# One core, attention feeding two expert layers: a new order of the front's queues, and its first fold row in plain fp32

## The reference

```python
# shortened; softmax stands for exp(s - max) / (sum + 1e-9)
def _attn_ref(x, state):                       # x (8, 8, 512, 64), state (8, 8, 32, 64)
    scores = scale * np.matmul(x, state.transpose(0, 1, 3, 2))
    a = softmax(scores)
    xread = np.matmul(a, state)
    scores2 = scale * np.matmul(state, x.transpose(0, 1, 3, 2))
    a2 = softmax(scores2)
    sread = np.matmul(a2, x)
    return np.concatenate([xread, sread], axis=2)
def _moe_ref(x, w1, w2, w3, w_out):            # d_model 512, d_ff 1024
    return ((x @ w1) * (x @ w2) @ w3) @ w_out
def _moe2_ref(x, w_in, w_out):                 # d_ff 2048
    h = x @ w_in
    return (h - np.tanh(h)) @ w_out
```

## Time and profile before

| | before |
|---|---|
| median of 3 runs | 1281.3 us (1281.1 to 1281.44) |
| profiled execution: its own time | 1281.57 us |
| its span, first to last instruction | 1279.8 us |
| PE busy | 1258.4 us, 98% of the span |
| PEld busy | 1015.4 us, 79% |
| DVE busy | 775.4 us, 61% |
| ACT busy | 555.0 us, 43% |
| POOL busy | 16.0 us, 1% |
| front: `scores(1)` starts | 20.22 us |
| front: `s1(0)` starts | 105.86 us |
| ys starts | 130.91 us |

### The profile page before, as it was taken

The page is one execution under the profiler, slowest core; times in us unless marked ns, Lnnn a source line. Parts: engine busy times, 40 slices in busy tenths (PEclk is TensorE's granted clock), DMA queues, the critical chain, the costliest instruction groups (busy, mean ns, idle before and its releaser), DMA issues.

```text
span 1279.8 us, 17464 instructions
## 1 busy us (share of the span) xinstructions
PE 1258.4 (98%) x6772; PEld 1015.4 (79%) x6772; DVE 775.4 (61%) x1269; ACT 555.0 (43%) x1034; POOL 16.0 (1%) x14
## 2 busy tenths in 40 slices
PE   8998999999999999999999999999999999999998
PEld 7777877777777777788888888888888888888887
DVE  6675244433333434678767677676676776776766
ACT  6675234323333333455444444444444344444443
POOL 0110000000000000000000000000000000000000
PEclk9999999999999999999999999999999999999999
DMA  9850200000000013212100100101001001010000
GB/s 376 309 188 1 83 1 33 34 1 34 34 1 33 34 34 115 66 50 67 50 1 17 50 9 9 50 18 49 0 16 49 0 17 49 16 35 7 8 34 17
DMA packets 17326, 63.77 MB, mean 50 GB/s; under 512 B 1904, under 2 KB 3056, under 8 KB 12656
## 3 DMA queue, kind: packets, MB, share of 16 engines
q1 hardware_dynamic: 16928, 62.59, 13.5%
q10 hardware_dynamic: 336, 0.33, 0.1%
HBM read 45.09 MB, written 17.83 MB: 49 GB/s over the span
## 4 chain that ended last, share of the span: by engine, by line
PE 57%; DVE 0%; ACT 0%; issue 0%; DVEq 0%
PE wide L1326 29%; PE bank L1304 28%; ACT ysb L1162 0%; DVE gsp_lo L1240 0%; DVE ysb L1292 0%; DVE gb L1269 0%; DVE hw L1250 0%; DVE gb L1257 0%; ACT gsp_hi L1176 0%; ACT hw L1188 0%; ACT hq L1183 0%; DVE gb L1267 0%; DVEq L1239 0%; DVEq L1255 0%
## 5 line engine op out<-in xcount | busy, mean ns | idle before, releaser
L1183 ACT ACTIVATE hq<-bank 128x512 f32<-128x512 f32 (+1 forms) x144 | 82.8, 575 | 397.9 <-PE bank L1304 397.8
L1304 PE MATMUL bank<-ysp_hi,wi_lo 128*128 128x512 f32 (+1 forms) x576 | 217.3, 377 | 0.0
L1304 PE MATMUL bank<-ysp_lo,wi_hi 128*128 128x512 f32 (+1 forms) x576 | 217.2, 377 | 0.0
L1304 PE MATMUL bank<-ysp_hi,wi_hi 128*128 128x512 f32 (+1 forms) x576 | 217.2, 377 | 0.0
L1326 PE MATMUL wide<-wz_hi,gsp_hi 128*128 128x512 f32 x544 | 212.6, 391 | 3.4 <-DVE gsp_lo L1240 2.5
L1250 DVE TENSOR_TENSOR hw<-hw,hq 128x512 f32<-128x512 f32 (+1 forms) x144 | 95.5, 663 | 196.8 <-ACT hw L1194 196.7
L1326 PE MATMUL wide<-wz_lo,gsp_hi 128*128 128x512 f32 x544 | 211.7, 389 | 0.0
L1326 PE MATMUL wide<-wz_hi,gsp_lo 128*128 128x512 f32 x544 | 211.7, 389 | 0.0
L1304 PEld LDWEIGHTS bank<-ysp_lo,wi_hi 128*128 128x128 f32 x576 | 108.4, 188 | 20.7
L1304 PEld LDWEIGHTS bank<-ysp_hi,wi_hi 128*128 128x128 f32 x576 | 108.2, 188 | 20.6
L1304 PEld LDWEIGHTS bank<-ysp_hi,wi_lo 128*128 128x128 f32 x576 | 108.2, 188 | 19.8
(11 more groups left out here) (123 smaller groups left out, 1772.1 us busy)
## 6 DMA issues: line engine op xcount, KB each, us to landing
xT<-in_x_cols SPq DMA_DIRECT2D x8, 1024.0 KB, 7.6
xs<-in_x_rows SPq DMA_DIRECT2D x8, 1024.0 KB, 5.0
y_dram<-ysb SPq DMA_DIRECT2D x8, 1024.0 KB, 4.3
out<-ysb SPq DMA_DIRECT2D x8, 1024.0 KB, 4.6
yr<-y_dram SPq DMA_DIRECT2D x28, 256.0 KB, 3.9
w3r<-in_w_cols SPq DMA_DIRECT2D x8, 512.0 KB, 5.7
w_raw<-in_moe_w SPq DMA_DIRECT2D x8, 512.0 KB, 9.1
wi_raw<-in_moe_w_in SPq DMA_DIRECT2D x4, 1024.0 KB, 7.1
```

The lines of the kernel that those rows point to most:

```text
L1183: act.activation(hq[:, f % 2, 0:w], ph[f % 2][:, 0:w], ACT.Square).then_inc(sq_done, 1)
L1304: mm = pe.matmul(ph[f % 2][:, 0:w], wi[s][c][:, f * P:(f + 1) * P], ysp[k][u][c][:, 0:w], start=c + m == 0, stop=c == KC - 1 and m == LAST)
```

## The change

The fold row 0 is taken out of the split scheme: four `first(n)` do it in plain fp32 from the tiles as loaded (`w3r[0]`, `wor`), 2 matmuls each in place of 6. The splits of w3 row 0 are gone, and w_out's low parts are written over `wor` only when `first` has read it. Each later entry takes the four pieces of row `r` = `e` and no others. The turn of the last entry's state reads stands behind the first piece, and `scores_turn` behind the second; `a2_turn` follows with one piece between it and `a_turn`. Both value units go behind `sread(7)`, the first of them into `pv` (the scores' banks). w_out's four parts are spread among other loads: x of batch 0 comes behind the first of them. The warm-up has 22 transposes. ACT and DVE orders are changed to suit, and ys starts its first two column blocks a product earlier.

```diff
-PIECES = (4, 5, 5, 4, 4, 4, 4, 2)
-WARM = 44
+WARM = 22
...
     def load_w3(eng, r):
-        after(eng, prod_done, r - 1)
+        if r == 2:
+            eng.wait_ge(first_done, 4)
+        else:
+            after(eng, prod_done, r - 2)
...
-        load_w3(sp, 0)
+        load_first(0)
         load_wo(0)
+        load_xT(sp, 0)
+        load_first(1)
         load_wo(1)
-        load_xT(sp, 0)
         load_wo(2)
+        load_xs(sp, 0)
         load_wo(3)
         load_w3(sp, 1)
-        load_xs(sp, 0)
...
# scalar (ACT)
+        split_wo(0)
+        copy_st(0)
         split_wo(1)
+        exp_a2(0)
         split_wo(2)
         turn_a2(0)
         exp_a(0)
-        pieces(0, 3)
+        split_w3(1)
         copy_sr(0)
+        split_wo(3)
+        empty_prod(0)
         for e in range(1, B):
             copy_st(e)
-            if e == 2:
-                split_w3(3)
+            if 1 < e < NF1 - 1:
+                split_w3(e + 1)
             if e >= B - WRING:
                 split_w(e - B + WRING)
-            pieces(e, 0)
             exp_a2(e)
-            pieces(e, 1)
+            turn_a(e - 1)
             if e == 1:
                 split_w3(2)
-            turn_a(e - 1)
+            turn_a2(e)
+            empty_prod(e)
             exp_a(e)
-            turn_a2(e)
-            pieces(e, 3, 4)
-            if 4 <= e + 2 < NF1:
-                split_w3(e + 2)
             copy_sr(e)
...
# vector (DVE)
         for e in range(1, B):
+            tokens_max(e)
             copy_srT(e - 1)
-            tokens_max(e)
+            if e == 1:
+                split_wo(3)
+            if 1 < e < NF1 - 1:
+                split_w3(e + 1)
             rows_max(e)
             rows_sub(e)
             tokens_invert(e)
...
+            if e >= B - WRING:
+                split_w(e - B + WRING)
+            empty_prod(e)
             rows_sum(e)
             rows_invert(e)
...
# tensor (PE)
+        def first(n):
+            pe.wait_ge(first_in[min(n, 1)], 16)
+            pe.wait_ge(wo_in[n], 16)
+            for k in (2 * n, 2 * n + 1):
+                mm = pe.matmul(pz[0], w3r[0][:, k, :], wor[:, k, :], start=k == 0, stop=k == NF1 - 1)
+            mm.then_inc(first_done, 1)
...
         warm()
+        first(0)
         scores(0)
         scores_turn(0)
-        piece(0, 2)
+        first(1)
         a2_turn(0)
-        piece(0, 3)
+        first(2)
         sread(0)
+        first(3)
         for e in range(1, B):
             scores(e)
+            piece(e, 0)
             sread_turn(e - 1)
-            piece(e, 0)
+            piece(e, 1)
             scores_turn(e)
-            piece(e, 1)
             a_turn(e - 1)
             piece(e, 2)
-            if e == B - 1:
-                pe.wait_ge(prod_lo, NF1)
-                values.tensor_unit(pe, 0, 0, pz)
             a2_turn(e)
-            if PIECES[e] > 3:
-                piece(e, PIECES[e] - 1)
+            piece(e, 3)
             sread(e)
-        pe.wait_ge(v_lo, 2)
+        values.tensor_unit(pe, 0, 0, pv)
+        sread_turn(B - 1)
+        pe.wait_ge(prod_lo, NF1)
         values.tensor_unit(pe, 0, 1, pz)
-        sread_turn(B - 1)
...
# s1(f): f == 1 waits for v_lo 2; ys: f == 0 waits for s1_pm NF1 - 1 (blocks 0, 1), then NF1 (blocks 2, 3)
-        pe.wait_ge(s1_pm, NF1)
+                if f == 0 and n % 2 == 0:
+                    pe.wait_ge(s1_pm, NF1 - 1 + n // 2)
```

More of the change, by code:

```diff
@@ L295, in stage_front @@
     w3_in, w3_hi, w3_lo = [sem(f"w3_in{n}") for n in range(2)], sem("w3_hi"), sem("w3_lo")
+    first_in, first_done = [sem(f"first_in{n}") for n in range(2)], sem("first_done")
     wo_in, wo_hi, wo_lo = [sem(f"wo_in{n}") for n in range(NF1 // 2)], sem("wo_hi"), sem("wo_lo")
@@ L307, in stage_front @@
     s1_done, s1_pm, s1_lo = sem("s1_done"), sem("s1_pm"), sem("s1_lo")
[L311 to L316, removed]
     def load_xT(eng, e):
@@ L379, in split_w3 @@
         def split_w3(r):
-            act.wait_ge(w3_in[r % 2], 16 * (r // 2 + 1))
-            after(act, prod_done, r - 1)
+            act.wait_ge(w3_in[r % 2], 16 * ((r + 1) // 2))
+            if r == 2:
+                act.wait_ge(first_done, 4)
+            else:
+                after(act, prod_done, r - 2)
             act.activation(w3T[0][r % 2][:, :, :], w3r[r % 2][:, :, :], ACT.Copy).then_inc(w3_hi, 1)
@@ L389, in empty_prod @@
         def empty_prod(r):
-            act.wait_ge(prod_done, r + 1)
+            if r == 0:
+                act.wait_ge(first_done, 4)
+            else:
+                act.wait_ge(prod_done, r)
             act.activation(w34[0][:, r, :], pz[r % 2], ACT.Copy).then_inc(prod_hi, 1)
[L393 to L396, removed]
         def split_w(f):
@@ L494, in scalar @@
             if f == 1:
+                values.scalar_unit(act, 0, 1, pz)
+            if f == 2:
                 turn_a(B - 1)
@@ L510, in empty_prod @@
             dve.tensor_tensor(w34[1][:, r, :], pz[r % 2], plain(w34[0][:, r, :]), ALU.subtract).then_inc(prod_lo, 1)
[L512 to L515, removed]
         def split_w(f):
@@ L574, in vector @@
         tokens_invert(0)
+        split_wo(0)
+        split_wo(1)
+        rows_sum(0)
         split_w3(1)
-        rows_sum(0)
-        pieces(0, 3)
         rows_invert(0)
+        split_wo(2)
+        empty_prod(0)
         for e in range(1, B):
+            tokens_max(e)
             copy_srT(e - 1)
-            tokens_max(e)
[L582 to L586, removed]
+            if e == 1:
+                split_wo(3)
+            if 1 < e < NF1 - 1:
+                split_w3(e + 1)
             rows_max(e)
@@ L684, in sread_turn, with piece @@
             pe.transpose(ps[:, W:W + P], sr[:, :], ident[:, :]).then_inc(sr_turned, 1)
[L686 to L690, removed]
+        def first(n):
[4 more added lines that the diff above has]
+            mm.then_inc(first_done, 1)
+        def piece(r, n):
             if n == 0:
-                pe.wait_ge(w3_lo, r + 1)
+                pe.wait_ge(w3_lo, r)
                 after(pe, prod_lo, r - 1)
-            if r == 0:
+            if r == 1:
                 pe.wait_ge(wo_lo, n + 1)
@@ L706, in s1 @@
             after(pe, s1_pm, f - 1)
+            if f == 1:
+                pe.wait_ge(v_lo, 2)
             pe.wait_ge(w_lo, f + 1)
```

45 lines of the change are left out of this document (14 added, 31 removed).

## The result

The changed kernel takes 1283.75 us in the median of 7 runs (1282.2 to 1286.84), the kernel before 1281.28 us (1280.22 to 1281.94) beside it: a ratio of 1.0019, 95% interval 1.001 to 1.0028. It is slower by about as much as the bound of "within 0.2%", where 0.3% faster was forecast. The profiled execution took 1283.73 us by its own time. Among the runs the longer ones have the lower mean granted clock: 0.999 at 1282.2 us, 0.996 at 1286.84.

The account below looks back on a forecast made before the run. PE, busy 98% of the span, was taken as the bound, with everything behind ys moving whole. Terms 0 + 4.4 - 1.0 + 0.3 gave 3.7 us off: 1277.6 us, likeliest 1276.3 to 1278.9, 8 in 10 1273.2 to 1280.2.

Parts of the forecast that it names:

- Entry 0: no gain: Front up to scores(1): plain fp32 row 0 hidden behind the loads, scores(1) at 20.2 us as before, 0 us gained.
- The old stalls go: Entries 1 to 7: PE's earlier waits vanish, scores(1) to sread(7) 73.2 us, 8.7 us less, before the new stall.
- A new stall in its place: Entries 2 to 7: POOL holds tbias, delaying the srT copy and scores_turn; six stalls of 0.71 us, 4.3 us lost.
- Behind sread(7): From sread(7) to s1(0): 4.8 us where it was 3.8, so 1.0 us lost.
- I take everything behind ys as a block that moves whole: moe1 and moe2, unchanged and PE back to back, only shift with the start of ys, 130.91 us before.
- the slower one, the clock of TensorE: Rival: after the shorter warm-up PE stays at the slower pace through entry 0; 8.7 us lost, 1286.3 us; chance 0.04.
- The late w3 loads: Rival, entries 4 to 6: late w3 loads stop exp_a2, then a2_turn; 1279.4 us; chance 0.18, including a larger new stall.

Follow-up runs that it names:

- four edits, WARM 22: Changed kernel, 22 warm-up transposes, plus copy_srT(e-1) ahead of tokens_max(e), rows_invert(7) behind the srT splits, w3 row 0 in one load: 1275.92 us.
- The swap of two lines: Changed kernel with copy_srT(e-1) ahead of tokens_max(e) on DVE, as it was before: 1279.53 us, ratio 0.9983.
- WARM 14, 10 and 6: Warm-up transposes: 14 and 6 in the kernel before (44 there), 1284.63 and 1282.68 us; 10 in the changed kernel with all four edits, 1276.63 us.
- WARM 52: Changed kernel with 52 warm-up transposes in place of 22: 1282.32 us, ratio 1.0009.
- the kernel with the other edits in: Changed kernel with both DVE order edits and w3 row 0 in one load: 1275.92 us at 22 warm-up transposes, 1279.60 at 30, 1274.31 at 38.

## Why the prediction was wrong

Its sum was a gain of 3.7 us from the front on. SP's first store of y stands at 143.88 us where it stood at 143.14, 0.7 later and not 3.7 earlier (ys itself started 6 of its matmuls ahead of the last product, as forecast, so its own start is no like mark).

```profile
143.14 0.66 SPq L763 DMA_DIRECT2D y_dram<-ysb  x1
```

```profile
143.88 0.66 SPq L753 DMA_DIRECT2D y_dram<-ysb  x1
```

So 4.4 us are missing up to it, and 1.4 behind it. By its own steps:

- **Entry 0: no gain.** That the plain fp32 row costs nothing was right: its matmuls took 0.91 us each (0.9 forecast; 14.79 to 16.61 us for a pair) and PE still waited for xT(1). That xT(1) lands at 20.1 was wrong: issued at 9.85, it took 11.1 us, to 20.95. I took the rate of the queue from the order before and gave no price to the cut of w3's row 0, whose first quarter goes in packets of 1 KB: between 1 and 6 us there were 304 packets under 2 KB, where the kernel before and the one with the row in one piece have 176. In one piece, xT(1) landed at 20.05. That the cut is the cause is shown by the kernels with and without it; that the small packets are, is not. **0.8 us.**
- **The old stalls go.** Right: all of the earlier trace rows ahead of s1 are gone, and without the new stall scores(1) to sread(7) takes 73.46 us (four edits, WARM 22) against the 73.2 of the forecast.
- **A new stall in its place.** Right in its mechanism, place and number, and slightly too small: `tbias` lasted 0.90 us (0.72 in the earlier trace rows) and `scores_turn` waited for the copy six times. DVE in entry 5 of the changed kernel, and POOL beside it:

```profile
68.49 1.16 DVE L520 TENSOR_REDUCE tmax<-stS 128x2 f32<-128x1024 f32 x1
69.69 0.90 DVE L522 TENSOR_SCALAR tbias<-tmax 128x2 f32<-128x2 f32 x1
70.51 0.28 DVE L558 COPY srT<-wide 128x128 f32<-128x128 f32 x1
...
68.66 1.91 POOL L374 TENSOR_TENSOR a<-a,rinv 128x1024 f32<-128x1024 f32 x1 [9.57 <-DVE rinv L554]
```

  `tbias` ends as POOL's op does, at 70.6. The entries took 11.48 us where 11.3 was forecast, against 10.64 without the stall: 0.84 us each for 0.71. Scores(1) to sread(7) 78.48 for 77.5: **1.0 us.** The swap of two lines gave 4.2 us, the most of any single edit.
- **Behind sread(7).** The step that failed most in the front. It was sized at 4.8 us; 5.92 were measured. I had `rows_invert` ahead of the copy in DVE's queue, and had not asked what POOL's op, which it releases, does to the next DVE work: the four `srs_lo`. I had priced the very same collision for `tbias`, and did not look for its second victim. **1.1 us.** With `rows_invert` behind them it was 4.15 us. And behind the longer wait the clock fell, which no step of the sum had: from `s1(0)` to the first y store it took 38.46 us in place of 37.28, where 0.3 less was forecast. The price of the clock can be read by itself: from `s1(0)` to ys it is 25.87 us here, and 24.38 in the two kernels in which the clock held behind the same wait. **1.5 us.**
- **"I take everything behind ys as a block that moves whole."** The premise failed. The block moved by +0.73 us up to 800 us and by 2.16 at 1061: **1.4 us**, from the position of the loop.

0.8 + 1.0 + 1.1 + 1.5 + 1.4 is 5.8 us, and the profiled execution differs from its forecast by 1283.73 - 1277.9 = 5.8. The terms are those of one execution: the clock in particular falls in some executions of a kernel and not in others.

Of the rivals, the slower one, the clock of TensorE, had the right resource and the wrong place: entry 0 was not slow, its matmuls took 0.91 us, but the work behind a wait of 2.5 us ninety us later was. Its reading of the earlier trace rows was off in two ways, neither of which touched the sum. The counts there are of transposes that lie in a stretch, not of those that start in it: the starts are 0.21 us apart at first and 0.11 later, so the warm-up of 22 ended at 6.5 us and not at 5.0. And the pace doubles within 0.1 us of the first entry of the clock (5.61 us in the kernel before), so it was the clock: the 1.00 printed ahead of it is no reading. In the changed kernel that entry is at 6.39 us, as first(0) begins; the kernels with WARM 14, 10 and 6 show what a still shorter warm-up costs. The late w3 loads did not come. The Trainium skill, TensorE: Matmul & The Clock Gate, § Why this matters for your kernels, warns of idle gaps between bursts; I had weighed that for entry 0 alone. The trace agrees that a gap can do it: clock 0.50 behind gaps of 2.46 and 2.86 us. It is no certainty: behind the same 2.5 us with WARM 52 the clock held 1.00. It held too in the kernel with row 0 in one load, whose warm-up is that of the changed kernel:

```profile
104.63 0.35 PE L708 MATMUL wide<-srs_hi,w_hi 128*128 128x256 f32 x1 [2.47 <-DVE srs_lo L590]
...
105.00:107.00 2.00, 2.00 (x19) 2.00 (x19) 1.69 (x4) 0.00 (x0) 0.00 (x0) 1.00 0.00 0
```

And the runs of the changed kernel alone differ, from 0.996 to 1.000 in the mean. So it is a matter of the execution at least as much as of the kernel. What decides between the two stays open.

The Trainium skill, SBUF — State Buffer, § A bandwidth-pool intuition that's wrong (but worth ruling out), which I had cited for `tbias`, says that contention is a lock; the second case agrees: the first subtraction was held until POOL had ended and took 1.64 us for 0.43, and the three behind it lost nothing. The lock works both ways: POOL's op of entry 0, which takes 1.91 us elsewhere, took 2.77 in the changed kernel, started 0.17 us behind a DVE subtraction.

```profile
20.03 1.16 DVE L504 TENSOR_TENSOR wos_lo<-wor,wos_hi 128x1024 fp32r<-128x1024 f32 x1
...
20.20 2.77 POOL L374 TENSOR_TENSOR a<-a,rinv 128x1024 f32<-128x1024 f32 x1 [18.73 <-DVE rinv L554]
```

Of the instruction fetches, the Trainium skill, Advanced Engine Details and Errata, § ISA Cache, states a cache line of 16 KB or 256 instructions and 128 KB on TensorE. The 16 KB of a packet agree; no run here shows the size of the cache.

## What to carry to other kernels

When an op of POOL is moved, look at every DVE op on SBUF tiles that it now runs beside, not only the next one, and keep such pairs apart where PE waits for the result: a wait of 2.5 us can cost its own length and the clock besides. A stage that nobody touched need not move whole: where a loop with a long body follows the edit, compare the steps between its stores and the number of instruction packets, and try a few instructions more or less ahead of the loop before the edit itself is judged. Here, in the kernel with the other edits in, 8 warm-up transposes more cost 3.7 us, and 16 more gave 1.6. (The 5.6 us between the changed kernel with 22 and with 30 are not the loop's alone: in the traces 3.0 us of the difference lie ahead of it, behind an xT(1) that came at 22.5 us.) And look at where the trace's entries of the clock begin before a short warm-up is called harmless.

## What the runs showed that was not expected

- Band of positions: 59 packets and 1.0 to 6.4 us lost with 6827 to 6843 instructions of PE ahead of moe2, 41 packets and nothing lost with 6823 and fewer or 6859 and more, in the code of both kernels.
- A full-size plain fp32 matmul (128 by 128 by 512) runs as two instructions and takes 0.91 us.
- A subtraction of two SBUF tiles on DVE is held by POOL's op (2.65 us for four against 1.43) and holds POOL in turn (2.77 against 1.91); a reduction beside the same op is not hurt (1.16).
- One load of 512 KB cut in a quarter and three quarters, at the head of the queue, let the transfer of xT(1), several loads later, land 0.9 us later (20.95 against 20.05), through one straggler among its 16 parts.
- Whether the clock falls behind a wait of 2.25 to 2.5 us differs between executions with the same code there: 0.50 in the changed kernel, 1.00 with WARM 52 and with row 0 in one load.
- PE starts at half its pace (transposes 0.21 us apart, then 0.11), and with a warm-up of 14, 10 or 6 transposes it stays there until 11.9 to 14.2 us.
